# Rows moved directly within SBUF, ahead of inputs and weights, with a later gate for four weight blocks and no empty output products

## The chip, the cores and the metric

The kernel runs on one core of a Trainium2 chip. The metric is the device time of one execution in microseconds (us); lower is better. The engines are TensorE (PE, with its weight loads PEld), VectorE (DVE), ScalarE (ACT), GpSimd (POOL) and SyncE (SP), which here only issues DMA transfers and waits.

## The reference

Three stages run one after the other on 4 batches x 768 tokens:

```
# 1. decaying linear attention, 8 heads of 48, one step per token
scale = minimum(|a|, 0.999) / (|a| + 1e-6);  a_n = a * scale          # a = a_re + i*a_im
S_re, S_im = a_n.re*S_re - a_n.im*S_im + outer(k_t, v_t),  a_n.re*S_im + a_n.im*S_re
y_t = q_t @ S_re
# 2. first network, 384 -> 1536 -> 384, 3072 tokens
xn = x / rms(x) * rms_g;   x1 = (silu(xn @ w_gate) * (xn @ w_val)) @ w_out
# 3. second network, 384 -> 2048 -> 384
out = softplus(x1 @ w_in) @ w_out2
```

## The kernel before

**Units and tiles.** The attention is cut into 24 units of 128 tokens. For unit n, ACT and DVE prepare decay factors, scaled keys and scaled queries (the steps named in `DVE_PREP`, from "t" to "Q") and write them into `pk`, which holds 384 rows (head and channel) as three blocks of 128 partitions, for the real and imaginary plane. The last of these DVE steps is "Q". TensorE needs the same rows in `mm`: partition = plane x channel (96), then head. The networks work on tiles of 512 tokens, four units each; there are six.

**From `pk` to `mm`.** A row of 257 numbers changes its partition on the way, so it goes through DRAM: `store_pk(n)` (L352) waits for step "Q" of unit n and writes all of `pk` to `rows_scratch`; `load_mm(m, hf)` (L345) waits for the store and reads four heads (half `hf`) back in two DMAs, one for each plane. Then `decay` (L1066, DVE) and `kt_of`, `scores`, `outputs` (PE) use them. `pk` is a single buffer: `decay_column(n)` on DVE, its first writer, waits until unit n-1 has left it.

**Three stages in time.** In the *lead* (units 0 to 5) no network runs. SP, ACT, DVE and PE each have a function `lead`, called once for each unit n: DVE prepares n, while the attention of unit m = n-1 and the norm of unit x = n-2 run beside it. Two of the first network's twelve weight blocks are also loaded in each: SP loads three slabs at a time into `ytile` (`load_w1`, L358), ACT writes a rounded copy and its negative (`w1_hi`, L647 and L649), POOL adds the original by an accumulating DMA (`w1_lo`, L518). Then the *first network* runs, six tiles of four steps; each step has three blocks of gate, value and output products on PE (L1488) and, beside them, the attention of one unit and the preparation of another. From unit 24 on there is nothing to prepare. The *second network* is products alone, with ACT and DVE for softplus.

**What sets the order.** Each engine runs its instructions in the order of the code, and only semaphores tie engines together. SP's order in the lead is: the a-input of unit n+1, values and rows of unit m, first weight block, keys and queries of n, second weight block, store of n:

```
load_a(n + 1)                     # waits for DVE step "an" of n
load_v(m); load_mm(m, 0, 1 - par); load_mm(m, 1, 1 - par)
load_w1(w1[0]); load_kq(n); load_w1(w1[1])
store_pk(n, par)                  # waits for DVE step "Q" of n
```

The a-input feeds `front_sq(n+1)` (ACT, L575), which comes in ACT's `lead(n)` after `products_by_row(n)`, and whose result `sum_of(n+1)` (DVE, L886) adds; that DVE instruction stands in `lead(n)` right after `after_sums(n, 1)`, ahead of the rest of unit n's own preparation. `load_v(m)` and the rows of half 1 wait until the attention of unit m-1 has used the buffers (`ys_done[1]`), the rows of half 0 for `ys_done[0]`.

Between lead and first tile PE waits for `y_copied`, `s_added`, all 36 `w_hi` and all 36 `w_lo`, and runs three products of a zero operand into `ybank` (L1636) that open an accumulation. The output products of a tile's last two blocks are put off into the next tile (`spill`), so tile 0 begins with two spills of a tile that doesn't exist: their operand is zero.

Of the kernel before, what the change touches and what calls it, by code (L numbers as in the profile page):

```python
# [18 lines left out]
F32 = mybir.dt.float32  # L19
F32R = mybir.dt.float32r  # L20
I32 = mybir.dt.int32
ALU = mybir.AluOpType
# [3 lines left out]
P = 128  # L26
B, H, S, D = 4, 8, 768, 48
DM = H * D
# [12 lines left out]
HH = H // 2  # L41
ROW = 2 * CH + 1
LEAD = 6
LAG = 1

SUM_LIMIT = -2000.0
# [83 lines left out]
def program(nc, a_d, kq_d, v_d, w1_d, w2_d, g_d, fa_d, fv_d, out_d):  # L130
    ctx = ExitStack()
    with ctx:
# [6 lines left out]
        def sem(name):  # L139
            return ctx.enter_context(nc.semaphore(name))  # L140


        rows_d = nc.dram_tensor("rows_scratch", (2, 2, DM, ROW), F32, kind="Internal").ap()
        y_d = nc.dram_tensor("y_scratch", (NT + 1, P, NJ, TOK), F32, kind="Internal").ap()

        x_d = nc.dram_tensor("x_scratch", (UNITS_B, BK, NBK, NE * B * H * EQ), F32, kind="Internal").ap()
# [70 lines left out]
        const_gp, const_ready = sem("const_gp"), sem("const_ready")  # L217
        gain_in, mask_out, mask_in = sem("gain_in"), sem("mask_out"), sem("mask_in")
        a_loaded, kq_loaded, v_loaded = sem("a_loaded"), sem("kq_loaded"), sem("v_loaded")
        pk_stored, mm_loaded = sem("pk_stored"), [sem(f"mm_loaded{i}") for i in range(2)]  # L220
        afront, aprep = Stage(sem("act_front"), ACT_FRONT), Stage(sem("act_prep"), ACT_PREP)
        s_done = sem("s_done")
        dprep = Stage(sem("dve_prep"), DVE_PREP)
# [3 lines left out]
        ys_done, y_copied, s_added, decayed = [sem(f"ys_done{i}") for i in range(2)], sem("y_copied"), sem("s_added"), sem("decayed")  # L227
        xt_done, xh_done, xl_done = sem("xt_done"), sem("xh_done"), sem("xl_done")
        w_loaded = [sem(f"w_loaded{i}") for i in range(3)]
        w_hi, w_neg, w_lo = sem("w_hi"), sem("w_neg"), sem("w_lo")  # L230
        w2_loaded = [sem(f"w2_loaded{i}") for i in range(3)]
        w2_hi, w2_lo = sem("w2_hi"), sem("w2_lo")
        gv_done, silu_done, p_done = sem("gv_done"), sem("silu_done"), sem("p_done")
# [87 lines left out]
        def _(sp):  # L321
# [16 lines left out]
                after((ys_done[1], m))  # L338
                sp.dma_start(v_in[:, :, :], v_d[m]).then_inc(v_loaded, 16)

            def load_mm(m, hf, par):
                after((pk_stored, 16 * (m + 1)), (ys_done[hf], m))
                heads = slice(hf * HH, (hf + 1) * HH)
                for z in range(2):
                    sp.dma_start(mm[z * D:(z + 1) * D, heads, :],  # L345
                                 rows_d[par, z].rearrange("(h d) c -> d h c", d=D)[:, heads, :]).then_inc(
                                     mm_loaded[hf], 16)

            def store_pk(n, par):

                after((dprep.sem, dprep.at("Q", n)))
                sp.dma_start(rows_d[par].rearrange("z (j p) c -> p z j c", p=P), pk[:, :, :, :]).then_inc(pk_stored, 16)  # L352

            def load_w1(f):
                for kind in range(3):
# [11 lines left out]
                    sp.dma_start(stage2[:, i, :], w2_d[f, kind]).then_inc(w2_loaded[i], 16)  # L367

            def lead(n, m, par, w1):
                load_a(n + 1)  # L370
                if m is not None:
                    load_v(m)
                    load_mm(m, 0, 1 - par)
                    load_mm(m, 1, 1 - par)
                load_w1(w1[0])
                load_kq(n)
                load_w1(w1[1])
                store_pk(n, par)

            def step(n, m, par):  # L380
                if m is not None:
                    load_v(m)
                    load_mm(m, 0, 1 - par)
                if n is not None and not (isinstance(n, int) and n + 1 >= NU):
                    load_a(n + 1)
                if m is not None:
                    load_mm(m, 1, 1 - par)
                if n is not None:
                    load_kq(n)
                if n is not None:  # L390
                    store_pk(n, par)

            def store_y(T):
                after((y_act, 2 * (T + 1)), (y_dve, T + 1))
# [87 lines left out]
        def _(pool):  # L482
# [32 lines left out]
            def w1_lo(f):  # L515
                for kind in range(3):
                    pool.wait_ge(w_neg, 3 * f + kind + 4)
                    pool.dma_start(slab[:, 6 * f + 2 * kind + 1, :], w1_d[f, kind],  # L518
                                   accum_op=ALU.add).then_inc(w_lo, 16)

            def w2_lo_of(slot):
                q0 = sum(len(x) for x in W2_PLAN[:slot])
# [351 lines left out]
        def _(dve):  # L874
# [129 lines left out]
                tt(scaled[:, :, :], frame[:, :, :], gv[:, :].unsqueeze(1).broadcast_to([P, 2, NJ]), ALU.mult, "Cim", n)  # L1004

            def decay_column(n):
                need(dve, pk_stored, 16 * n)
                tick(dve.tensor_copy(pk[:, :, :, 2 * CH], carry[:, :].unsqueeze(1).broadcast_to([P, 2, NJ])))

            def last_products(n):  # L1010
# [49 lines left out]
                return pk[:, z, :, first:first + CH].rearrange("p j (i b) -> p j i b", i=BK)  # L1060

            def decay(m, hf):
                dve.wait_ge(mm_loaded[hf], 32 * (m + 1))
                need(dve, s_added, 2 * m + hf - 1)
                heads = slice(hf * HH, (hf + 1) * HH)
                dve.tensor_tensor(state[:, heads, :], state[:, heads, :],  # L1066
                                  mm[:, heads, 2 * CH:2 * CH + 1].broadcast_to([2 * D, HH, D]), ALU.mult).then_inc(decayed, 1)
# [416 lines left out]
        def _(pe):  # L1484
# [4 lines left out]
                return last  # L1489

            def kt_of(m, hf):
                pe.wait_ge(mm_loaded[hf], 32 * (m + 1))
                need(pe, y_copied, 2 * m + hf)
                need(pe, s_added, 2 * m + hf)
                for h in range(HH):
                    last = pe.transpose(xbank[:, h * 2 * D:(h + 1) * 2 * D], mm[:, hf * HH + h, 0:CH],  # L1496
                                        ident[0:2 * D, 0:2 * D])
                last.then_inc(kt_done, 1)
# [31 lines left out]

            def gate_val(T, f, par, kind):
                g = 2 * f + kind
                if kind == 0:
                    pe.wait_ge(p_done, F1 * T + f)
                else:
                    need(pe, silu_done, F1 * T + f + 1)
                for k in range(NJ):
                    last = split_product(gbank[g % 3][:, :], 6 * f + 2 * kind, slice(k * P, (k + 1) * P),
                                         xh[:, par, k, :], xl[:, par, k, :], k == 0, k == NJ - 1)
                last.then_inc(gv_done, 1)  # L1540
# [19 lines left out]
                last.then_inc(out_done, 1)  # L1560

            def out_block(T, f):
                if f < 2:
                    spill(T, f)
                else:
                    out_of(T, f - 2, f == 2, False)
# [35 lines left out]
            def lead(m, x):  # L1602
# [4 lines left out]
                        last = pe.transpose(lead_xt[:, j * CH:(j + 1) * CH], xn[:, j * P:(j + 1) * P], ident[:, :])  # L1607
                    last.then_inc(xt_done, 1)
                for hf in range(2):
                    pe.wait_ge(mm_loaded[hf], 32 * (m + 1))  # L1610
                    need(pe, y_copied, 2 * m - 1 + hf)
                    need(pe, s_added, 2 * m - 1 + hf)
                    for h in range(HH):
                        last = pe.transpose(lead_bank[hf][:, h * 2 * D:(h + 1) * 2 * D], mm[:, hf * HH + h, 0:CH],
                                            ident[0:2 * D, 0:2 * D])
                    last.then_inc(kt_done, 1)
                    need(pe, masked, 2 * m - 1 + hf)
                    for h in range(HH):
                        last = pe.matmul(lead_scores[hf][:, h * CH:(h + 1) * CH], mm[:, hf * HH + h, 0:CH],
                                         mm[:, hf * HH + h, CH:2 * CH], start=True, stop=True)  # L1620
                    last.then_inc(sc_done, 1)
# [6 lines left out]
                lead(m, m - 1)  # L1628
            pe.wait_ge(y_copied, 2 * (LEAD - 1))
            pe.wait_ge(s_added, 2 * (LEAD - 1))  # L1630
            pe.wait_ge(w_hi, 3 * F1)
            pe.wait_ge(w_lo, 16 * 3 * F1)
            pe.wait_ge(silu_done, 1)

            for m in range(NJ):
                pe.matmul(ybank[m][:, :], slab[:, 0, 0:P], ph[:, 0, :], start=True, stop=False)  # L1636
            for T in range(NT):
                tile(T, T % 2)

# [92 lines left out]


CONSTS = 17
W1_LEAD = [(2 * n, 2 * n + 1) for n in range(LEAD)]
W2_RANK = [i for slot in W2_PLAN for i in range(len(slot))]

# [43 lines left out]
```

## Time and profile before

| | |
|---|---|
| Three runs | 1174.2 us median (1171.81 to 1175.09) |
| Profiled execution | 1175.1 us; span from first to last instruction 1173.4 us |
| PE / DVE / ACT / POOL busy | 1074.7 / 701.8 / 679.3 / 290.2 us |
| Lead, up to the store of unit 5 | 0 to 148.9 us |
| First network from its first product | 156.5 to about 766 us |
| DMA moved | 98.15 MB |

In the profile, a line such as L345 is that of kernel.py. "Idle before, releaser" is how long an engine stood still ahead of an instruction and what ended it. SPq rows are DMA issues: the start is when SP began to issue, the duration is that of the issue, and the time to landing is told separately.

### The profile page before, as it was taken

How to read it: one execution, taken by the hardware profiler on the slowest of the kernel's cores; microseconds unless marked ns; L12 is line 12 of the kernel's file. 1: busy time of each engine (PE TensorE's matmuls, PEld its weight loads, DVE VectorE, ACT ScalarE, POOL GpSimd, SP SyncE). 2: the span in 40 equal slices, each digit the busy share in tenths (PEclk: the TensorE clock that was granted, in tenths of full speed). 3: DMA queues.
4: the chain of work that ended last, by engine and by line, in shares of the span. 5: the costliest groups of instructions: out<-in, count | busy, mean ns of one | idle time of the engine just before them, and what ended most of it. 6: DMA issues, size and time to landing. Idle time of an engine off the chain costs nothing.

```text
span 1173.4 us, 17259 instructions
## 1 busy us (share of the span) xinstructions
PE 1074.7 (92%) x5495; PEld 913.2 (78%) x5495; DVE 701.8 (60%) x2227; ACT 679.3 (58%) x1217; POOL 290.2 (25%) x260
## 2 busy tenths in 40 slices
PE   0456689999999999999999999989999999999997
PEld 0456678888888888888888878878888888888886
DVE  7798959999999999999999211212221313122211
ACT  5566646555555565665554333466666667676664
POOL 2211211111111111111111116733333333333332
PEclk9999999999999999999999999989999999999999
DMA  4988853433343443334332303320100101010000
GB/s 114 208 206 216 189 128 88 115 89 88 89 137 100 106 132 107 88 88 116 88 89 75 101 1 122 119 70 1 52 3 1 55 0 54 0 54 0 27 1 28
DMA packets 69051, 98.15 MB, mean 84 GB/s; under 512 B 5232, under 2 KB 58864, under 8 KB 68976
## 3 DMA queue, kind: packets, MB, share of 16 engines
q1 hardware_dynamic: 63792, 90.15, 27.0%
q0 software_dynamic: 5184, 7.08, 3.9%
q8 instruction: 38, 0.62, 0.2%
q14 instruction: 37, 0.30, 0.1%
HBM read 67.97 MB, written 29.24 MB: 83 GB/s over the span
## 4 chain that ended last, share of the span: by engine, by line
PE 34%; issue 26%; DVE 11%; DMA 11%; POOL 10%; ACT 6%; SPq 1%; POOLq 0%; DVEq 0%; ACTq 0%
PE gbank L1488 16%; POOL pl L556 10%; PE ybank L1488 10%; DMA rows_scratch<-pk 5%; DMA mm<-rows_scratch 4%; DVE prep L882 3%; PE sbank L1505 2%; DVE pk L882 2%; PE xbank L1517 2%; PE xbank L1516 1%; PE xbank L1520 1%; ACT L730 1%; PE xbank L1496 1%; DMA ytile<-in_w 1%; DVE state L1066 1%
## 5 line engine op out<-in xcount | busy, mean ns | idle before, releaser
L1488 PE MATMUL gbank<-xh,slab 128*128 128x512 f32 x1296 | 404.3, 393 | 1.5 <-ACT xh L641 1.5
L1488 PE MATMUL ybank<-ph,slab 128*128 128x512 f32 x1020 | 319.6, 395 | 4.8 <-ACT ytile L678 3.9
L1488 PEld LDWEIGHTS gbank<-xh,slab 128*128 128x128 f32 x1296 | 241.5, 189 | 50.2 <-ACT xh L641 1.7
L1488 PE MATMUL gbank<-xl,slab 128*128 128x512 f32 x648 | 253.3, 391 | 0.0
L1488 PEld LDWEIGHTS ybank<-ph,slab 128*128 128x128 f32 x1020 | 189.3, 189 | 42.9 <-issue 5.6
L531 POOL TENSOR_TENSOR pl<-hid,ph 128x512 fp32r<-128x512 f32 x72 | 99.7, 1384 | 461.4 <-ACT ph L671 461.4
L1488 PE MATMUL ybank<-pl,slab 128*128 128x512 f32 x510 | 199.6, 391 | 0.0
L556 POOL TENSOR_TENSOR pl<-hid,ph 128x512 fp32r<-128x512 f32 x96 | 125.6, 1309 | 268.0 <-ACT ph L817 268.0
L1368 DVE SCALAR_TENSOR_TENSOR hid<-gbank,hid 128x512 f32<-128x512 f32 x72 | 49.7, 691 | 214.4 <-ACT hid L808 214.4
L1488 PEld LDWEIGHTS gbank<-xl,slab 128*128 128x128 f32 x648 | 122.0, 188 | 26.2
L1488 PEld LDWEIGHTS ybank<-pl,slab 128*128 128x128 f32 x510 | 96.2, 189 | 20.8
L671 ACT ACTIVATE ph<-hid 128x512 fp32r<-128x512 f32 x72 | 45.8, 637 | 105.7 <-PE ybank L1488 100.9
L1136 DVE TENSOR_TENSOR hid<-gbank,hid 128x512 f32<-128x512 f32 x72 | 49.4, 686 | 90.1 <-PE gbank L1488 90.0
L817 ACT ACTIVATE ph<-hid 128x512 fp32r<-128x512 f32 x96 | 60.6, 631 | 72.4 <-DVE hid L1368 70.3
L882 DVE TENSOR_TENSOR prep<-prep 128x384 f32<-128x384 f32 (+2 forms) x264 | 88.9, 367 | 1.7
L1516 PE MATMUL xbank<-v_in,at 128*128 128x48 f32 x344 | 68.7, 283 | 8.1 <-issue 6.6
L1517 PE MATMUL xbank<-state,mm 96*128 96x48 f32 x344 | 71.3, 291 | 0.0
L808 ACT ACTIVATE hid<-hid,one 128x512 f32<-128x512 f32 x96 | 69.4, 723 | 3.2
L666 ACT ACTIVATE hid<-gbank 128x512 f32<-128x512 f32 x72 | 42.7, 592 | 44.0 <-PE gbank L1488 43.1
L1516 PEld LDWEIGHTS xbank<-v_in,at 128*128 128x128 f32 x344 | 58.2, 207 | 11.0 <-issue 9.4
L804 ACT ACTIVATE hid<-gbank 128x512 f32<-128x512 f32 x72 | 43.0, 597 | 39.6 <-PE gbank L1488 39.6
L1368 DVE SCALAR_TENSOR_TENSOR hid<-xbank,hid 128x512 f32<-128x512 f32 x24 | 16.6, 692 | 81.8 <-ACT hid L808 81.8
(155 smaller groups left out, 1604.0 us busy)
## 6 DMA issues: line engine op xcount, KB each, us to landing
rows_scratch<-pk SPq DMA_DIRECT2D x24, 771.0 KB, 4.9
mm<-rows_scratch SPq DMA_DIRECT2D x96, 192.8 KB, 4.5
a_in<-in_a SPq DMA_DIRECT2D x24, 384.0 KB, 4.9
kq_in<-in_kq SPq DMA_DIRECT2D x24, 384.0 KB, 5.9
ytile<-in_w SPq DMA_DIRECT2D x36, 192.0 KB, 4.7
slab<-in_w POOLq DMA_DIRECT2D x36, 192.0 KB, 5.7
prep<-in_w SPq DMA_DIRECT2D x32, 192.0 KB, 2.5
y_scratch<-ytile SPq DMA_DIRECT2D x7, 768.0 KB, 5.4
```

Source lines behind the costliest of these rows:

```text
L531: pool.tensor_tensor(pl[:, f % 2, :], hid[:, f % 2, :], ph[:, f % 2, :].bitcast(F32), ALU.subtract).then_inc(lo_done, 1)
L556: pool.tensor_tensor(pl[:, f % 2, :], hid[:, f % 2, :], ph[:, f % 2, :].bitcast(F32), ALU.subtract).then_inc(lo2_done, 1)
L671: act.activation(ph[:, f % 2, :], hid[:, f % 2, :], ACT.Copy).then_inc(hi_done, 1)
L804: act.activation(hid[:, f % 2, :], hbank[f % 4][:, :], ACT.Abs).then_inc(abs_done, 1)
L808: act.activation(hid[:, f % 2, :], hid[:, f % 2, :], ACT.Ln, bias=one[:, 0:1]).then_inc(l_done, 1)
L817: act.activation(ph[:, f % 2, :], hid[:, f % 2, :], ACT.Copy).then_inc(hi2_done, 1)
L882: tick(dve.tensor_tensor(out, a, b, op))
L1136: dve.tensor_tensor(hid[:, f % 2, :], gbank[(2 * f + 1) % 3][:, :], hid[:, f % 2, :], ALU.mult).then_inc(p_done, 1)
L1368: dve.scalar_tensor_tensor(out=hid[:, f % 2, :], in0=hbank[f % 4][:, :], scalar=0.0, in1=hid[:, f % 2, :], op0=ALU.max, op1=ALU.add).then_ ...
L1488: last = pe.matmul(out, slab[:, slot + part, cols], x, start=f, stop=l)
L1516: pe.matmul(bank[:, h * D:(h + 1) * D], at[:, h, :], v_in[:, head, :], start=True, stop=False)
L1517: pe.matmul(bank[:, h * D:(h + 1) * D], mm[:, head, CH:2 * CH], state[:, head, :], start=False, stop=True)
```

## The change

`rows_scratch`, `store_pk` and `load_mm` are gone. `move_rows(m, hf)` copies straight from `pk` to `mm` within SBUF. A head's 48 rows lie in one or two of `pk`'s blocks, so a half has five pieces (heads 2 and 5 have two each), and with two planes ten DMAs, 20 for a unit. In the lead the moves, which wait for step "Q" of unit n-1, stand ahead of the a-input of unit n+1 and the weights; in a tile's step they take the place of the loads. `decay_column` waits for both halves' moves of the unit before. PE waits for 24 `w_hi` and `w_lo` (eight blocks) before tile 0, and for the others at block 8 of tile 0. The zero products now end their accumulation, they signal `out_done` by 2, and the two spills of tile 0 are left out.

```
+EARLY = 8
-            def load_mm(m, hf, par):
-                after((pk_stored, 16 * (m + 1)), (ys_done[hf], m))
-                heads = slice(hf * HH, (hf + 1) * HH)
+            def move_rows(m, hf):
+                after((dprep.sem, dprep.at("Q", m)), (ys_done[hf], m))
                 for z in range(2):
-                    sp.dma_start(mm[z * D:(z + 1) * D, heads, :],
-                                 rows_d[par, z].rearrange("(h d) c -> d h c", d=D)[:, heads, :]).then_inc(
-                                     mm_loaded[hf], 16)
-            def store_pk(n, par):
-                after((dprep.sem, dprep.at("Q", n)))
-                sp.dma_start(rows_d[par].rearrange("z (j p) c -> p z j c", p=P), pk[:, :, :, :]).then_inc(pk_stored, 16)
+                    for h, d, j, p, rows in PIECES[hf]:
+                        sp.dma_start(mm[z * D + d:z * D + d + rows, h, :], pk[p:p + rows, z, j, :]).then_inc(mm_loaded[hf], 16)
...
             def lead(n, m, par, w1):
+                if m is not None:
+                    move_rows(m, 0)
+                    load_v(m)
+                    move_rows(m, 1)
                 load_a(n + 1)
-                if m is not None:
-                    load_v(m)
-                    load_mm(m, 0, 1 - par)
-                    load_mm(m, 1, 1 - par)
                 load_w1(w1[0])
                 load_kq(n)
                 load_w1(w1[1])
-                store_pk(n, par)
             def step(n, m, par):
                 if m is not None:
                     load_v(m)
-                    load_mm(m, 0, 1 - par)
+                    move_rows(m, 0)
                 if n is not None and not (isinstance(n, int) and n + 1 >= NU):
                     load_a(n + 1)
                 if m is not None:
-                    load_mm(m, 1, 1 - par)
+                    move_rows(m, 1)
                 if n is not None:
                     load_kq(n)
-                if n is not None:
-                    store_pk(n, par)
...
             def decay_column(n):
-                need(dve, pk_stored, 16 * n)
+                need(dve, mm_loaded[0], MOVED * n)
+                need(dve, mm_loaded[1], MOVED * n)
...
             def gate_val(T, f, par, kind):
+                if T == 0 and f == EARLY and kind == 0:
+                    pe.wait_ge(w_hi, 3 * F1)
+                    pe.wait_ge(w_lo_late, 16 * 3 * (F1 - EARLY))
             def out_block(T, f):
+                if T == 0 and f < 2:
+                    return
...
-            pe.wait_ge(w_hi, 3 * F1)
-            pe.wait_ge(w_lo, 16 * 3 * F1)
+            pe.wait_ge(w_hi, 3 * EARLY)
+            pe.wait_ge(w_lo, 16 * 3 * EARLY)
             for m in range(NJ):
-                pe.matmul(ybank[m][:, :], slab[:, 0, 0:P], ph[:, 0, :], start=True, stop=False)
+                last = pe.matmul(ybank[m][:, :], slab[:, 0, 0:P], ph[:, 0, :], start=True, stop=True)
+            last.then_inc(out_done, 2)
...
+def pieces(hf):
+    out = []
+    for h in range(hf * HH, (hf + 1) * HH):
+        d = 0
+        while d < D:
+            c = h * D + d
+            rows = min(D - d, P - c % P)
+            out.append((h, d, c // P, c % P, rows))
+            d += rows
+    return out
+PIECES = [pieces(hf) for hf in range(2)]
+MOVED = 16 * 2 * len(PIECES[0])
```

## Rows read from the trace of the kernel before

**Rows 1.** Windows: stretch, length, busy us (instructions) of each engine, clock, DMA share, GB/s
```profile
126.04:148.91 22.87, 15.53 (x77) 14.73 (x77) 21.49 (x84) 15.02 (x33) 4.71 (x6) 1.00 0.89 213
...
370.00:477.00 107.00, 105.63 (x625) 90.79 (x624) 102.43 (x350) 62.54 (x118) 16.98 (x12) 1.00 0.38 104
```

**Rows 2.** Timeline of SP, lead and tile 0: start, duration, queue, line, destination<-source, count
```profile
21.30 2.26 SPq L358 DMA_DIRECT2D ytile<-in_w x3
27.96 0.39 SPq L352 DMA_DIRECT2D rows_scratch<-pk  x1
28.39 5.30 SPq L421 DMA_DIRECT2D causal<-mask_scratch  x8
...
52.93 0.38 SPq L352 DMA_DIRECT2D rows_scratch<-pk  x1
...
101.60 0.38 SPq L352 DMA_DIRECT2D rows_scratch<-pk  x1
106.58 0.33 SPq L330 DMA_DIRECT2D a_in<-in_a  x1
...
107.53 2.07 SPq L345 DMA_DIRECT2D mm<-rows_scratch  x4
...
126.04 0.38 SPq L352 DMA_DIRECT2D rows_scratch<-pk  x1
...
130.62 0.33 SPq L339 DMA_DIRECT2D v_in<-in_v  x1
...
148.91 0.38 SPq L352 DMA_DIRECT2D rows_scratch<-pk  x1
...
188.24 0.39 SPq L352 DMA_DIRECT2D rows_scratch<-pk  x1
```

**Rows 3.** Source view of L345 (ns min/median/max); DMA view, 28 to 157 us
```profile
L345 SPq DMA_DIRECT2D mm<-rows_scratch x96: 303/410/550, 35.0 to 650.9; - x96
...
a_in<-in_a SPq DMA_DIRECT2D x5, 384.0 KB, 4.6
```

**Rows 4.** Waits of DVE, 28 to 149 us: total, times, longest
```profile
DVE prep L910 <- ACT prep L593: 6.7, 4, 2.5
DVE state L1066 <- DMA mm<-rows_scratch: 4.6, 7, 1.0
```

**Rows 5.** Timelines of DVE and ACT in the lead, around the sum
```profile
110.86 0.84 ACT L575 ACTIVATE front<-a_in 128x768 f32<-128x768 f32 x1 [0.89 <-DMA a_in<-in_a]
...
112.62 0.55 DVE L886 TENSOR_TENSOR front<-front 128x384 f32<-128x384 f32 x1
...
135.54 0.55 DVE L886 TENSOR_TENSOR front<-front 128x384 f32<-128x384 f32 x1
```

**Rows 6.** Timelines of DVE and PE where the first tile begins
```profile
153.86 0.35 DVE L1079 TENSOR_TENSOR state<-gbank,state 96x192 f32<-96x192 f32 x1 [1.88 <-ACT xnat L690]
...
156.52 1.62 PE L1636 MATMUL ybank<-ph,slab 128*128 128x512 f32 x3 [3.06 <-DMA slab<-in_w]
...
160.50 1.05 PE L1488 MATMUL gbank<-xh,slab 128*128 128x512 f32 x2
...
163.14 0.62 PE L1488 MATMUL gbank<-xh,slab 128*128 128x512 f32 x2
...
164.09 0.69 DVE L1136 TENSOR_TENSOR hid<-gbank,hid 128x512 f32<-128x512 f32 x1 [9.41 <-PE gbank L1488]
```

**Rows 7.** Chain of waits: start, duration, what (one block of output products)
```profile
182.09 2.08 PE ybank L1488 x9
```

**Rows 8.** Timelines of DVE and PE in a step of the first network
```profile
415.23 0.56 DVE L886 TENSOR_TENSOR front<-front 128x384 f32<-128x384 f32 x1 [0.30 <-ACT front L575]
...
421.76 0.52 PE L1496 MATMUL xbank<-ident,mm 96*128 96x96 f32 x4 [0.19 <-DVE state L1101]
```

**Rows 9.** Waits of PE, 157 to 690 us
```profile
PE xbank L1496 <- DVE state L1101: 4.0, 11, 0.7
...
PE xbank L1496 <- DMA mm<-rows_scratch: 2.4, 5, 0.9
```

More of the change, by code:

```diff
@@ L140, in sem @@
             return ctx.enter_context(nc.semaphore(name))
-        rows_d = nc.dram_tensor("rows_scratch", (2, 2, DM, ROW), F32, kind="Internal").ap()
         y_d = nc.dram_tensor("y_scratch", (NT + 1, P, NJ, TOK), F32, kind="Internal").ap()
@@ L219, in program @@
         a_loaded, kq_loaded, v_loaded = sem("a_loaded"), sem("kq_loaded"), sem("v_loaded")
-        pk_stored, mm_loaded = sem("pk_stored"), [sem(f"mm_loaded{i}") for i in range(2)]
+        mm_loaded = [sem(f"mm_loaded{i}") for i in range(2)]
         afront, aprep = Stage(sem("act_front"), ACT_FRONT), Stage(sem("act_prep"), ACT_PREP)
@@ L229, in program @@
         w_loaded = [sem(f"w_loaded{i}") for i in range(3)]
-        w_hi, w_neg, w_lo = sem("w_hi"), sem("w_neg"), sem("w_lo")
+        w_hi, w_neg, w_lo, w_lo_late = sem("w_hi"), sem("w_neg"), sem("w_lo"), sem("w_lo_late")
         w2_loaded = [sem(f"w2_loaded{i}") for i in range(3)]
@@ L518, in w1_lo @@
                     pool.dma_start(slab[:, 6 * f + 2 * kind + 1, :], w1_d[f, kind],
-                                   accum_op=ALU.add).then_inc(w_lo, 16)
+                                   accum_op=ALU.add).then_inc(w_lo if f < EARLY else w_lo_late, 16)
             def w2_lo_of(slot):
@@ L1062, in decay @@
             def decay(m, hf):
-                dve.wait_ge(mm_loaded[hf], 32 * (m + 1))
+                dve.wait_ge(mm_loaded[hf], MOVED * (m + 1))
                 need(dve, s_added, 2 * m + hf - 1)
@@ L1491, in kt_of @@
             def kt_of(m, hf):
-                pe.wait_ge(mm_loaded[hf], 32 * (m + 1))
+                pe.wait_ge(mm_loaded[hf], MOVED * (m + 1))
                 need(pe, y_copied, 2 * m + hf)
@@ L1609, in lead @@
                 for hf in range(2):
-                    pe.wait_ge(mm_loaded[hf], 32 * (m + 1))
+                    pe.wait_ge(mm_loaded[hf], MOVED * (m + 1))
                     need(pe, y_copied, 2 * m - 1 + hf)
```

## The prediction

> **What bounds the kernel now.** I read the windows first, to cut the run into stages, then for each stage the timeline of the engine that is nearly full, then SP's timeline, because the change is mostly one of SP's order. In the lead DVE is busy 21.5 of 22.9 us of a unit while PE has 15.5 and the DMA share is 0.89; in the first network DVE has 102.4 and PE 105.6 of 107 us [rows 1]. So in the lead the time is DVE's list plus what DVE stands still for; in the first network DVE and PE hold each other, and neither has 5% to give.
>
> The length of a lead unit is the distance between two stores, since each store waits for DVE's last step "Q": units 1 to 5 take 148.91 - 27.96 = 120.95 us, and the four from 52.93 on take 95.98, or 24.0 each [rows 2]. In these five units DVE waits 6.7 us for ACT at L910 (ACT is late there because it converts weights first) and 4.6 us for `mm` at L1066 [rows 4]. For the a-input it hardly waits: ACT squares it at 110.86, 9.3 us after the store at 101.60, and DVE adds it at 112.62, 11.0 after that store [rows 2, 5].
>
> **The moves in the lead.** Removed: one store and four loads of a unit. Added: 20 issues on SP, in the same place in time (right after "Q"), and everything that SP issues later in that unit stands behind them. Let Q be the time of the last unit's step "Q". What does an issue cost? L345's median is 0.41 us, 0.30 at the least and 0.55 at most [rows 3]; four in a row take 2.07, 0.52 each, and eight transfers of only 8 KB take 5.30, 0.66 each with one long one among them [rows 2]. So small pieces are not cheaper to issue than large ones. I take 0.445 from one start to the next: the median issue, and a little for the gap between two. The ends that I keep are 0.36 and 0.50.
>
> - Ten moves of half 0: Q to Q+4.45. The values then wait for `ys_done[1]`, which before let them go 4.58 us after the store (130.62 - 126.04) [rows 2]; that is now Q+4.6, and they take 0.35.
> - Ten moves of half 1: Q+4.95 to Q+9.4. Only now is the a-input issued, at Q+9.4. Before it was Q+5.0 (106.58 - 101.60) [rows 2].
> - It lands 4.6 us later, the median of the lead's five [rows 3] (ends 3.5 and 5.8 for other traffic around it): Q+14.0. The square takes 0.84 [rows 5], with the signal 0.9: DVE can add at Q+14.9, where before it added at Q+11.0.
> - From that instruction to the next "Q", DVE needed 148.91 - 135.54 = 13.37 and 126.04 - 112.62 = 13.42 us [rows 2, 5]. Of this the waits for `mm` go away, since the last move is issued by Q+9.4 and even at the 4.6 of a larger transfer has landed by Q+14: 4.6 / 5 = 0.9 each [rows 4]. That leaves 12.5.
>
> A lead unit thus takes 14.9 + 12.5 = 27.4 us against 24.0: four of them 109.6 - 95.98 = **+13.6**. The 6.7 us for ACT at L910 are no gain, as that stall lies ahead of the sum, where DVE now has slack. Unit 1 is reckoned apart. SP's last weight issue before it ends at 23.56; the eight mask loads no longer stand behind a store and take 5.3, to 28.9; moves and values take 9.3, to 38.2; landing, square and the rest give 38.2 + 4.6 + 0.9 + 12.5 = 56.2 for the second "Q", which was at 52.93 [rows 2]: **+3.3**. The lead: **+16.9**. What else is behind the moves has room: keys and queries are issued near Q+11.5 and used some 7 us after the sum, the first weight block is needed after the ACT work that follows the square. DRAM traffic of the rows falls away (0.77 MB each way), and that helps landings, not issues.
>
> With the ends: 0.36 and 3.5 us give an a-input issued at Q+8.6, a sum at Q+13.0 and units of 25.5, so +6.0 in four and nothing in unit 1, **+6**. With 0.50 and 5.8 it is Q+10.4, Q+17.1 and 29.6, +22.4 and some 5 in unit 1, **+28**.
>
> On small transfers the Trainium skill speaks against the change: "DMA: Bandwidth & Descriptors", section "Rules for kernel authors", says to coalesce many small transfers, because under 64 KB one pays mostly overhead. The trace agrees as far as issues go, 0.66 us each for 8 KB against 0.52 for 193 KB [rows 2]. By the page's fit in its section on the SWDGE path (2.0 us plus bytes / 436e3) a piece of 49 KB would be estimated at 2.1 us; if the 20 pieces of a unit ran strictly one after the other, that would be 42 us a unit, longer than a whole step. But the eight 8 KB loads were issued inside 5.3 us, so issues at least overlap what the page puts into one transfer.
>
> **The start of tile 0.** PE waited 3.06 us for the last weight slab and began at 156.52 [rows 6]. The new gate of eight blocks is long open; what is late next is the state add at 153.86 + 0.35 = 154.2 [rows 6], 5.3 us after the last "Q" of the lead. That is **-2.3**, if the clock follows. The trace has two matmuls in 1.05 us at 160.50 and in 0.62 at 163.14 [rows 6]: PE started the tile at the lower of its two levels (1.2 GHz) and had the upper one some 5 us of unbroken work later. If the rise stays where it is in time and doesn't move with the start, the first products take longer and the gain is 0.8. I take -2.2. The last four blocks are awaited at block 8, more than two steps later, and four steps take 107 us [rows 1], so by then they have been there for about 50; this wait costs nothing and has nothing behind it.
>
> **No empty products.** PE loses 18 products and their weight loads; nine take 2.08 [rows 7], so that is 4.1 us of PE work, half of it directly after the first value product. But from 164.09, where that value product is ready, to the next "Q" at 188.24 [rows 2, 6] DVE needs 24.1 us, and its timeline shows it at work nearly without a break. The attention outputs need DVE's mask, and the keys of half 1 need its state add. PE, now earlier, will wait there instead: what was a product becomes a wait. I take **0**, with -4.1 as the other end.
>
> **The moves in the tiles.** A step is a ring: PE to ACT, ACT's square to DVE's sum (waited 0.30 at 415.23), DVE's state add to PE's keys (waited 0.19 at 421.76) [rows 8]. None of it passes through `mm`. The a-input there waits for DVE's "an", which follows the first gate product, so ten moves are through by about the same time; half 1 of the rows and the keys are issued some 2 us later than before, and both are used only near the end of the step. What is gained is at most PE's waits for `mm`, 2.4 us in five places [rows 9], some of which DVE (4.0 in eleven) takes over. I take **-1**, between -2.4 and 0. If this cover failed, each microsecond would count 18 times; half a microsecond each would be +9, inside the range. The wait in `decay_column` stands behind `decay(m, 1)`, which already waits for the same moves: nothing.
>
> **Sum.** +16.9 - 2.2 + 0 - 1 = +13.7. The profiled execution took 1175.1 us (span 1173.4 and 1.7 around it), so 1188.8; it lies 0.9 above the median of the three runs, against which the same sum gives 1187.9. I say **1188**. Its own range, from the ends, is +6 - 2.3 - 2.4 = +1 to +28 - 0.8 = +27 at the extremes, 1176 to 1202; both ends of every term together are unlikely.
>
> **Rivals.**
> - *Faster: the a-input is not late.* The five DVE waits for `mm` (4.6 us) and the start (2.2) are gained, and some of the empty products: -8 or so, **1166**. For it speaks that these waits stand in the profile, and that the rows' way is one transfer shorter. It decides at DVE's sum in the lead: for a unit no longer than 24.0 us the sum must come by Q+11.5 and the a-input be issued by Q+6, so 20 issues must take less than 5.5 us, under 0.28 each. The least of 96 issues is 0.30 [rows 3]. 12%.
> - *Near no change:* cheap issues and quick landings, with all of the gains at the start and at `mm`: +1, **1175.5**. 12%.
> - *The empty products count in full*, because PE and not DVE sets tile 0: 13.7 - 4.1, **1184**. Against it is DVE's full list there. 12%.
> - *The moves are slow as transfers too*, so that the a-input queues behind them: +27, **1202**. For it: DMA share 0.89 in the lead [rows 1]. Against: half of the rows' traffic goes away. 10%.
> - *The pieces run one after the other*, 2 us or so each, as the rule above would have it at its worst: 42 us a unit instead of 24 and 27, some +350 us, near **1520**. The eight mask loads speak against it. 2%.
> - The forecast: 52%.
>
> Slower by over 0.3% is the forecast, the third, fourth and fifth rivals and a little of the second: 0.77. Within 0.3% (3.5 us, about what these measurements can tell from no change) 0.10, faster 0.13. For eight in ten I take 1175 to 1200.
>
> **What would show it.** In the changed kernel's lead DVE should wait at L886 (the sum) for ACT, about 5 us for each of units 1 to 5, and ACT at the square for the a-input by as much; the waits at L910 matter no more and those for `mm` are gone; SP should show ten issues in about 4.5 us; the distance of two "Q" should be near 27.4. PE should begin tile 0 some 5.3 us after the last lead "Q", then wait for DVE in the first step; steps should stay at 26.7. I am wrong if DVE has no wait at its sum, or if the steps change.

## The result, and the profile of the changed kernel

The changed kernel takes **1202.8 us** (median of four runs, 1201.78 to 1204.25) against 1174.1 (1171.81 to 1175.09): the ratio is **1.0244, 95% interval 1.0226 to 1.0261**. Slower was forecast, but by 13.7 us and not by 28.7, and 1202.8 lies above the range of 1175 to 1200. The profiled execution took 1201.78 us with a span of 1200.0, so the spans differ by 26.6.

First the windows, for they say in which stage the time went. The columns are the stretch and its length, busy us (instructions) of PE, PEld, DVE, ACT and POOL, the granted clock, the DMA share and GB/s. A lead unit, and four steps of the first network, of the changed kernel:

```profile
118.86:148.98 30.12, 15.56 (x77) 14.84 (x77) 21.46 (x84) 15.03 (x33) 5.39 (x7) 1.00 0.58 137
401.00:508.00 107.00, 105.94 (x626) 90.81 (x624) 102.53 (x350) 62.45 (x119) 17.00 (x12) 1.00 0.26 75
```

Beside [rows 1] the same 84 instructions of DVE take the same 21.5 us in a lead unit, but the unit is 30.1 us long instead of 22.9 (over the five units 30.2 on average instead of 24.2). The DMA share fell from 0.89 to 0.58, so the lead got slower with less traffic. Four steps still fill 107 us. (The clock column reads 1.00 in the lead, but two of the attention's small matmuls take 0.63 us there, and 0.39 at 199.82 in the first step. So PE is at its lower level in the lead, in the kernel before too; there DVE and not PE sets the time.) Cut at the end of DVE's step "Q", the whole difference comes out as follows:

| Stretch | before | after | difference |
|---|---|---|---|
| Q of unit 0 to Q of unit 5 (five lead units) | 121.0 | 151.0 | +30.0 |
| to the next Q (the first tile begins in it) | 39.3 | 38.2 | -1.1 |
| the next 16 steps | 429.7 | 428.8 | -0.9 |
| the rest | 555.5 | 554.1 | -1.4 |

So the lead lost 30.0 us. The reason stands on SP's timeline (start, duration of the issues, queue, line, destination<-source, count):

```profile
88.88 6.23 SPq L345 DMA_DIRECT2D mm<-pk  x10
95.16 0.58 SPq L339 DMA_DIRECT2D v_in<-in_v  x1
95.83 6.22 SPq L345 DMA_DIRECT2D mm<-pk  x10
102.10 0.58 SPq L330 DMA_DIRECT2D a_in<-in_a  x1
...
118.86 6.27 SPq L345 DMA_DIRECT2D mm<-pk  x10
```

Ten moves start at Q (88.88), the values follow at once, and then ten more. From the first move to the values is 6.28 us, 0.63 for each issue. The a-input is issued 13.2 us after Q, where it was 5.0 before [rows 2]. What follows from it stands on ACT and DVE:

```profile
105.41 0.84 ACT L565 ACTIVATE front<-a_in 128x768 f32<-128x768 f32 x1 [8.25 <-DMA a_in<-in_a]
...
106.38 0.56 DVE L876 TENSOR_TENSOR front<-front 128x384 f32<-128x384 f32 x1 [6.48 <-ACT front L565]
```

ACT has stood still for 8.25 us when the a-input is there, and DVE for 6.48 when it may add. That add comes 17.5 us after Q, where it was 11.0 [rows 5], and the next Q is 118.86 - 106.38 = 12.5 us later. DVE's waits from 28 to 165 us (total, times, longest):

```profile
DVE front L876 <- ACT front L565: 30.8, 4, 8.6
DVE prep L900 <- ACT prep L583: 4.0, 5, 1.5
```

The waits for `mm` of [rows 4] are gone, those at the line that was L910 went from 6.7 to 4.0, and the new wait at the sum is 30.8 us in four of the five units (with the fifth, up to 179 us, 38.2).

The other place is the start of tile 0. PE's timeline (the number in brackets is how long PE had stood still, and for whom):

```profile
184.33 1.62 PE L1632 MATMUL ybank<-ph,slab 128*128 128x512 f32 x3 [0.85 <-ACT xnat L680]
...
199.82 0.39 PE L1507 MATMUL xbank<-v_in,at 128*128 128x48 f32 x2 [3.64 <-DVE at L1082]
...
204.74 1.05 PE L1479 MATMUL gbank<-xh,slab 128*128 128x512 f32 x2
...
208.30 0.62 PE L1479 MATMUL gbank<-xh,slab 128*128 128x512 f32 x2
```

PE begins 184.33 - 178.9 = 5.4 us after the last Q of the lead, as forecast (before: 156.52 - 148.91 = 7.6 [rows 6]). The 3.06 us for the weight slab are gone. But nine of the 18 empty products stood right ahead of the attention output (the other nine some 7 us earlier), and there PE now stands still for 3.64 us, waiting for DVE's mask. From 201 until about 208 us two matmuls take 1.05 us instead of the 0.62 that they take at the end, and DVE has to wait for one of the gate products among them. DVE's wait, and the window (columns as above):

```profile
209.95 0.69 DVE L1127 TENSOR_TENSOR hid<-gbank,hid 128x512 f32<-128x512 f32 x1 [2.03 <-PE gbank L1479]
```

```profile
199.50:210.00 10.50, 10.18 (x46) 8.86 (x47) 8.37 (x46) 5.94 (x10) 1.29 (x1) 0.67 0.16 48
```

The granted clock was 0.67 there, a mix of the two levels, 1.2 and 2.4 GHz. DVE is busy 8.37 of the 10.50 us.

### The profile page after: what moved, and what is told of

Its sections match the earlier page's. It is cut to its first block, busy times and chain, and to the rows that moved or that the text cites. A ratio compares the mean times of both kernels' runs of the same rounds, so it can differ in the third digit from the quotient of the medians.

```text
span 1200.0 us, 17585 instructions
## 1 busy us (share of the span) xinstructions
PE 1071.9 (89%) x5477; PEld 912.3 (76%) x5477; DVE 701.5 (58%) x2227; ACT 678.2 (57%) x1217; POOL 290.8 (24%) x260
## 3 DMA queue, kind: packets, MB, share of 16 engines
q1 hardware_dynamic: 51120, 71.22, 19.7%
## 4 chain that ended last, share of the span: by engine, by line
PE 35%; issue 27%; DVE 10%; POOL 10%; ACT 10%; DMA 5%; SPq 2%; POOLq 0%; DVEq 0%; ACTq 0%
PE gbank L1479 17%; POOL pl L546 10%; PE ybank L1479 10%; DVE prep L872 3%; DMA ytile<-in_w 3%; SPq L345 2%; PE xbank L1508 2%; PE xbank L1507 2%; DMA a_in<-in_a 2%; PE sbank L1496 2%; ACT L720 2%; ACT front L565 2%; PE xbank L1511 1%; ACT prep L599 1%; PE xbank L1487 1%
## 5 line engine op out<-in xcount | busy, mean ns | idle before, releaser
L1479 PE MATMUL ybank<-ph,slab 128*128 128x512 f32 x1008 | 315.9, 395 | 4.8 <-ACT ytile L668 3.9
L1479 PE MATMUL ybank<-pl,slab 128*128 128x512 f32 x504 | 197.0, 391 | 0.0
L1479 PEld LDWEIGHTS gbank<-xl,slab 128*128 128x128 f32 x648 | 122.3, 189 | 26.2
L508 POOL DMA_DIRECT2D slab<-in_w x36 | 30.9, 860 | 148.2 <-ACT slab L639 147.1
L794 ACT ACTIVATE hid<-gbank 128x512 f32<-128x512 f32 x72 | 43.0, 597 | 39.6 <-PE gbank L1479 39.6
```

What stands on the lines that cost most here:

```text
L794: act.activation(hid[:, f % 2, :], hbank[f % 4][:, :], ACT.Abs).then_inc(abs_done, 1)
L1479: last = pe.matmul(out, slab[:, slot + part, cols], x, start=f, stop=l)
```

## The experiments

Four kernels at first, beside a kernel before at 1174.43 us. The theory was that the time sits in the lead, because the a-input stands behind twenty slow issues.

**a_between.** The a-input goes out between the two rows of ten; nothing else changes.

```diff
                 if m is not None:
                     move_rows(m, 0)
+                load_a(n + 1)
+                if m is not None:
                     load_v(m)
                     move_rows(m, 1)
-                load_a(n + 1)
```

> The changed kernel with one thing moved: in the lead, SP issues the a-input after the ten moves of half 0 instead of after all twenty. Theory (the lead is long because DVE waits for the a-input, which stands behind twenty issues of 0.62 us): the a-input is issued near Q+6.3 and DVE's sum comes by Q+11; the moves of half 1 end some 0.6 us later, near Q+13.6, so DVE waits 1 to 2 us for them; a lead unit takes 24 to 25 us instead of 30, and the time is 1173 to 1180. Rival (the moves themselves or their transfers slow the lead, wherever the a-input stands): the units stay near 30 and the time at 1200 or more.

Measured: 1183.13 us (1182.96 to 1185.11), ratio 1.0074 (1.0047 to 1.0101). One reordering takes back 19.7 of the 28.7 us. SP and DVE in one unit:

```profile
81.37 6.23 SPq L345 DMA_DIRECT2D mm<-pk  x10
87.64 0.58 SPq L330 DMA_DIRECT2D a_in<-in_a  x1
```

```profile
91.88 0.56 DVE L877 TENSOR_TENSOR front<-front 128x384 f32<-128x384 f32 x1 [0.93 <-ACT front L566]
...
96.46 0.35 DVE L1058 TENSOR_TENSOR state<-state,mm 96x192 f32<-96x192 f32 x1 [2.29 <-DMA mm<-pk]
```

The a-input is issued 6.3 us after Q, the sum comes at Q+10.5, and the wait there shrinks to 0.93. Units are 26.2 to 26.9 us long instead of 29.7 to 31.3. They don't reach 24, since now the second row of moves is late: DVE waits 2.29 us for it, 11.2 us in the five units. A third wait is new, 4.7 us in the five units for the keys and queries: SP issues them 15.3 us after Q as in the changed kernel, but DVE now comes to them sooner. The time is 3 us above the upper end of what I had expected, for I had not reckoned the second wait so high, nor the third at all.

**dram_source.** The same twenty pieces, of the same shape, read from an input in DRAM instead of from `pk`. The attention thus works on wrong rows; the order of the work is unchanged.

```diff
-  sp.dma_start(mm[...], pk[p:p + rows, z, j, :])
+  sp.dma_start(mm[...], kq_d[m][p:p + rows, z, 0:ROW])
```

> The changed kernel, but each of the twenty pieces of a unit is read from rows of the key input in DRAM, of the same count, length and partitions, instead of from pk; so the attention works on wrong rows, and only the time counts. Theory A (an issue costs 0.62 us instead of 0.45 because both ends are in SBUF): issues fall to about 0.45, lead units to about 27, the time to about 1187. Theory B (a row of ten small issues costs 0.62 each whatever the source): issues and units stay as they are, time 1200 to 1205.

Measured: 1185.50 us (1183.02 to 1186.93), ratio 1.0088 (1.0060 to 1.0116). SP in one unit:

```profile
81.61 4.55 SPq L345 DMA_DIRECT2D mm<-in_kq  x10
86.21 0.42 SPq L339 DMA_DIRECT2D v_in<-in_v  x1
86.73 4.56 SPq L345 DMA_DIRECT2D mm<-in_kq  x10
91.33 0.42 SPq L330 DMA_DIRECT2D a_in<-in_a  x1
```

The count, the sizes and the destination are the same, only the source is not: ten issues take 4.55 instead of 6.23 us, 0.46 instead of 0.63 from start to start. Units are 25.9 to 27.7, where 27.4 was forecast. With about the issue cost that the forecast had taken (0.46 for 0.445) the unit comes out close to the forecast, 26.7 on average. The issue of the values and of the a-input behind the moves costs 0.42 here too, and 0.58 in the changed kernel.

**a_late.** The kernel before, with the a-input issued behind the four loads of rows. Nothing else of the change is in it, and it has few issues.

```diff
             def lead(n, m, par, w1):
-                load_a(n + 1)
                 if m is not None:
                     load_v(m)
                     load_mm(m, 0, 1 - par)
                     load_mm(m, 1, 1 - par)
+                load_a(n + 1)
```

> The kernel before the change, rows through DRAM, with the a-input of the lead issued after the four loads of rows instead of ahead of them: near Q+8 instead of Q+5. Theory (the place of the a-input sets the unit): DVE's sum comes at about Q+13.5 and units take 26 us instead of 24, so the time is 1182 to 1186. Rival (DVE has slack for the a-input): no change, 1174.

Measured: 1188.12 us (1187.25 to 1189.98), ratio 1.0110 (1.0076 to 1.0145). SP in one unit, and DVE's largest wait from 28 to 165 us:

```profile
90.08 1.78 SPq L345 DMA_DIRECT2D mm<-rows_scratch  x4
91.91 0.44 SPq L330 DMA_DIRECT2D a_in<-in_a  x1
```

```profile
DVE front L886 <- ACT front L575: 22.5, 5, 4.9
```

A late a-input alone, with four issues ahead of it, makes the kernel 13.7 us slower, and it shows in the very wait of the changed kernel. That is what the theory says of the mechanism. The units (26.6 to 28.2) are longer than expected, and the time is 2 us above the range. The clock isn't what makes them so: the column gives 0.59 from 54.5 to 164.6 us here (0.70 in dram_source, 1.00 in the changed kernel), but two of the attention's matmuls take 0.63 us in the lead of all three, and the two executions of a_late with a mean clock of 0.998 took 1187.25 and 1188.49 us.

**empty_kept.** The changed kernel with the 18 empty products put back. They read blocks 0 and 1, which the early gate covers, so that the gate stays early.

```diff
             def out_block(T, f):
-                if T == 0 and f < 2:
-                    return
 ...
```

> The changed kernel with the eighteen empty output products of tile 0 put back (with weight blocks 0 and 1, whose product with zero is the same). Theory (without them PE stands still 3.6 us before the attention outputs of the first step, its clock falls to the lower level and the next products take twice as long, which costs DVE 2 us at its third gate product): PE has no wait there, no matmul in the step runs at the lower level, and the time is about 2 us lower, 1200.8 against 1202.8. Rival (fewer products are a gain or nothing): the time is the same or up to 4 us higher.

Measured: 1201.07 us (1200.98 to 1201.36), ratio 1.0224 (1.0189 to 1.0258): 1.75 us *faster* than without those products, by the medians. The intervals of the two ratios overlap, but the slowest of its four runs is below the fastest of the changed kernel's (1201.78). PE at the places of the third fence of the result:

```profile
200.57 0.32 PE L1507 MATMUL xbank<-v_in,at 128*128 128x48 f32 x2
...
203.73 0.62 PE L1479 MATMUL gbank<-xh,slab 128*128 128x512 f32 x2
```

and the same window:

```profile
199.50:210.00 10.50, 9.82 (x64) 8.45 (x63) 10.07 (x49) 8.03 (x14) 1.29 (x1) 1.00 0.17 51
```

There is no wait ahead of the output, the clock is 1.00, and the two matmuls take 0.62. PE gets through 64 instructions in the 10.5 us instead of 46. The stretch from the last Q of the lead to the next one is 36.3 us instead of 38.2.

The other kernels bear this out. From DVE's first gate product to the next Q it takes 24.1 or 24.2 us in all eight that keep the products, with a clock of 1.00 in these 10.5 us of the step. In the four that leave them out (the changed kernel, a_between, dram_source, hybrid_no_empty) PE waits 3.64 or 3.65 us ahead of the output, the clock is 0.54 to 0.67, and the stretch takes 26.1 to 27.1 us.

The second set asks whether there is a version that keeps the gains and not the cost. It stands beside a kernel before at 1175.04 us.

**gate_only.** The kernel before with the later gate for the last four blocks alone; the empty products stay and read blocks 0 and 1.

```diff
-            pe.wait_ge(w_hi, 3 * F1)
-            pe.wait_ge(w_lo, 16 * 3 * F1)
+            pe.wait_ge(w_hi, 3 * EARLY)
+            pe.wait_ge(w_lo, 16 * 3 * EARLY)
...
+                if T == 0 and f == EARLY and kind == 0:
+                    pe.wait_ge(w_hi, 3 * F1)
+                    pe.wait_ge(w_lo_late, 16 * 3 * (F1 - EARLY))
```

> The kernel before the change with only the late gate for the last four weight blocks (the empty products stay, with blocks 0 and 1). Theory: TensorE begins tile 0 about 5 us after the lead's last Q instead of 7.5, nothing else moves, and the time falls by 2 to 3 us, to about 1172. Rival (the clock rises later or DVE is late anyway): no change, 1174.

Measured: 1171.87 us (1168.68 to 1175.21), ratio 0.9977 (0.9964 to 0.9991). PE begins the tile 5.4 us after the last Q (148.87), 2.2 earlier than in [rows 6]:

```profile
154.30 1.62 PE L1640 MATMUL ybank<-ph,slab 128*128 128x512 f32 x3 [0.85 <-ACT xnat L691]
...
157.98 0.63 PE L1489 MATMUL gbank<-xh,slab 128*128 128x512 f32 x2
```

Two matmuls take 0.63 us already at 157.98, 3.7 after PE's start; before they took 1.05 still at 160.50, 4.0 after it, and had had a wait of 3.06 us ahead [rows 6]. So the clock rises sooner too. From that Q to the next it takes 36.2 us instead of 39.3: the 2.2 of the earlier start and about 0.9 on top.

**tiles_direct.** The kernel before with the direct moves in the tile steps only; the lead keeps its way through DRAM.

```diff
             def lead(n, m, par, w1):
 ...
-                store_pk(n, par)
+                if n < LEAD - 1:
+                    store_pk(n, par)
             def step(n, m, par):
 ...
-                    load_mm(m, 0, 1 - par)
+                    move_rows(m, 0)
```

> The kernel before the change with the direct moves in the tiles' steps only; in the lead the rows still go through DRAM. Theory (twenty issues of 0.63 us a unit fit beside a step of 26.7 us, and mm is there a little earlier): the distance of two Qs stays at 26.7 and the time is 0 to 2.5 us lower, 1172 to 1174. Rival (half 1 or the keys come late in the steps): steps grow, 1178 or more.

Measured: 1171.97 us (1168.94 to 1175.06), ratio 0.9978 (0.9967 to 0.9990). PE's waits in the tiles, 157 to 690 us:

```profile
PE xbank L1505 <- DVE state L1110: 5.9, 17, 0.8
```

The 2.4 us for `mm` of [rows 9] are gone, and DVE has taken over a part of them, 5.9 us where it was 4.0. The 16 steps take 428.8 us instead of 429.7, and the stretch ahead of them 37.7 instead of 39.3.

**hybrid.** Both together: gate_only's edits and those of tiles_direct.

> Both of these together: rows through DRAM in the lead, direct in the tiles, late gate, empty products kept. If the parts add: 4 to 5 us below the kernel before, 1169.5, with lead units at 24. If the gain at the start is taken back by DVE in the first steps: 1172 to 1174.

Measured: **1171.29 us** (1167.99 to 1172.99), ratio **0.9972 (0.9961 to 0.9983)**. It beats both kernels: 0.3% under the one before, 2.6% under the changed one. Its last lead unit, with the 21.6 us of DVE's work and the high DMA share of [rows 1], is 24 us long and not 30:

```profile
123.33:147.29 23.96, 15.60 (x77) 14.80 (x77) 21.58 (x84) 15.14 (x33) 5.73 (x7) 1.00 0.91 208
```

The two parts gained 3.2 and 3.1 us alone and 3.75 together, which leaves hybrid about 2 us above what I had expected. In the profiles both shorten the same stretch: the one that holds the last lead Q to the next (36.2 and 37.7 us alone, 36.6 together, 39.3 before). So they overlap there, and by the intervals hybrid isn't shown to be faster than either part alone.

**act_a.** The changed kernel, but ACT issues the a-input of the lead, so no move is ahead of it. Two things more differ: on SP the keys and queries go ahead of the first weight block, and the empty products are kept.

```diff
             def lead(n, m, par, w1):
 ...
                     move_rows(m, 1)
-                load_a(n + 1)
-                load_w1(w1[0])
                 load_kq(n)
+                load_w1(w1[0])
 # in ACT's list, after the middle of unit n
+                act.dma_start(a_in[:, :, :], a_d[n + 1]).then_inc(a_loaded, 16)
```

> The changed kernel with the a-input of the lead issued by ACT right after its step that waits for the same DVE step, the keys ahead of the weights on SP, and the empty products kept; all twenty moves stay where the change put them. Theory (of the moves only their being ahead of the a-input costs time): lead units fall from 30 to 24.5 to 26, bounded by the last of twenty moves at Q+12.8 plus 2 us of landing, and the time is 1170 to 1178. Rival (twenty issues cost the lead 6 us a unit however the a-input comes): units near 30, 1200.

Measured: 1175.57 us (1174.17 to 1176.35), ratio 1.0004 (0.9991 to 1.0017). SP in one unit of the lead, and DVE at the state's decay in it:

```profile
102.84 6.24 SPq L345 DMA_DIRECT2D mm<-pk  x10
109.80 6.23 SPq L345 DMA_DIRECT2D mm<-pk  x10
```

```profile
118.19 0.35 DVE L1057 TENSOR_TENSOR state<-state,mm 96x192 f32<-96x192 f32 x1 [2.48 <-DMA mm<-pk]
```

SP issues the same twenty dear moves, at the same price, and the time is 27.3 us below the changed kernel's, of which the empty products are some 1.8 (empty_kept). So it was not the moves that cost most of the time, but that the a-input stood behind them; a_between shows the same with the a-input's place alone, where here the keys moved too. The units are 24.5 to 25.9 us, and the lead takes 126.5 us where it was 121.0: what is left is that the last of the twenty moves is late (9.5 us of waits in four units). The gains behind the lead make up for it.

The last two ran beside a kernel before at 1175.42 us.

**store_split.** The kernel before with its one store cut into six of 128 rows each, so that the issue of a piece from SBUF to DRAM can be read.

```diff
-                sp.dma_start(rows_d[par].rearrange("z (j p) c -> p z j c", p=P), pk[:, :, :, :]).then_inc(pk_stored, 16)
+                for z in range(2):
+                    for j in range(NJ):
+                        sp.dma_start(rows_d[par][z, j * P:(j + 1) * P, :], pk[:, z, j, :]).then_inc(pk_stored, 16)
```

> The kernel before the change with the store of a unit's rows cut into six (one for each plane and block of 128 partitions), to measure one thing, the distance of two issues in a row whose source is SBUF and whose destination is DRAM. Theory A (reading from SBUF makes an issue dear): 0.63 us, as for the moves. Theory B (only SBUF at both ends does): 0.46 us, as for loads from DRAM. The time is some 2 to 3 us a lead unit higher in A and 1.5 to 2 in B, as the loads wait for the last store.

Measured: 1195.47 us, a single run. SP:

```profile
28.20 2.79 SPq L354 DMA_DIRECT2D rows_scratch<-pk  x6
```

Six issues in 2.79 us are 0.47 each: with the source in SBUF and the destination in DRAM an issue costs about what it does the other way round. Of the kinds tried, only pieces with both ends in SBUF cost 0.63. The lead's five units grew by 4.3 us, 0.9 each and not the 1.5 to 2 expected. The run is 20 us slower all the same, which I had not expected, because the rows arrive later in every tile step: from 240 to 600 us PE waits 13.4 us for `mm` in 13 places, where it was 1.6 in 4, and 16 steps take 444.4 us instead of 429.7, 27.8 each instead of 26.9. SP issues the rows' loads 1.2 to 1.7 us later after Q, so their way through DRAM has less than a microsecond of room in a tile step.

**hybrid_no_empty.** hybrid with the empty products taken out.

> The hybrid (rows through DRAM in the lead, direct in the tiles, late gate) with the eighteen empty products of tile 0 left out too. Theory (without them TensorE stands still before the first attention outputs and falls to the lower clock): a wait of 3 to 4 us there, matmuls at half speed after it, the distance from the lead's last Q to the next 1 to 2 us longer than the hybrid's 36.6, and the time 1172 to 1173. Rival (4.1 us less work for TensorE is a gain once the lead is short): 1168 to 1170.

Measured: 1174.04 us (1170.39 to 1176.18), ratio 0.9982 (0.9966 to 0.9997). PE:

```profile
171.63 0.63 PE L1526 MATMUL xbank<-v_in,at 128*128 128x48 f32 x2 [3.65 <-DVE at L1101]
...
177.74 1.05 PE L1498 MATMUL gbank<-xh,slab 128*128 128x512 f32 x2
...
181.04 0.62 PE L1498 MATMUL gbank<-xh,slab 128*128 128x512 f32 x2
```

The same wait of 3.65 us and the same matmuls at the lower level appear in a kernel whose lead is not slow, and the stretch from Q to Q is 39.6 us instead of 36.6. So it is the missing products and nothing else of the change that brings them. In the profile it is 3 us; by the ratios, with hybrid's beside it, 0.001 or 1.2 us, and those intervals overlap. The sign is borne out by two pairs of kernels and by the stretch of all twelve profiles; what it is worth in the time of the whole kernel, 1 to 3 us, isn't settled.

## Why the prediction was right and wrong

**The mechanism was right.** DVE waits for ACT at its sum, ACT for the a-input, the next Q is 12.5 us after the sum (12.5 forecast), the steps kept their length, and a_between and a_late move the time by moving the a-input alone. The size was half of what came.

**The step that failed is the cost of an issue in "the moves in the lead".** The text asked "What does an issue cost?" and took 0.445 us, with 0.36 and 0.50 as its ends. It measured 0.63, above the upper end. The a-input was thereby issued at Q+13.2 and not at Q+9.4, +3.8 us a unit. Its landing was quicker than taken, 3.4 us (median of the lead's five) for 4.6: -1.2. That the rows' traffic had halved doesn't explain it, for in act_a, with the same moves, the a-input takes 4.6 again. The sum so came at Q+17.5 for Q+14.9. The four units from the second Q on took 30.3 on average for 27.4, +11.7, and the second Q itself came at 57.6 for 56.2, +1.4: that is the missing 13.1 us of the lead (+30.0 for +16.9). The rows that I took the price from [rows 3] have one end in DRAM, as all transfers of SP in that profile. For a transfer with both ends in SBUF the trace of before had no row, and the ends of the range were those of a different kind of transfer. I named the 0.66 for each of eight mask loads [rows 2] and then left it outside the range. It would have given the right number, but by luck. The same eight loads in the changed kernel:

```profile
23.59 3.87 SPq L411 DMA_DIRECT2D causal<-mask_scratch  x8
```

That is 0.48 each, so a small size alone doesn't make an issue dear, and the prediction's reading that 8 KB cost more to issue than 193 KB doesn't hold.

**Where SBUF lies at both ends, and not how many rows a piece has**, decides the price. Pieces of 16, 32 and 48 rows had issues of 0.59 us each (medians) in the changed kernel, and dram_source kept the pieces and changed the source.

**The start of tile 0** was forecast as -2.2. From the last Q to PE's first product it gained 2.2 (7.6 to 5.4), and gate_only shows it by itself. DVE's first gate product came 12.0 us after Q, where it was 15.2: 3.2, because the clock came up sooner too: two matmuls took the full 1.05 us for the last time at 185.75, 1.4 us after PE's start, where it was 4.0 after it before. The end of the term that said the rise might stay where it is in time was wrong; it moved forward by more than the start.

**The empty products** were forecast as 0 with -4.1 as the other end, and the text said "what was a product becomes a wait". The wait came (3.64 us for 4.1 us of products), and the text stopped there. A wait is not as good as a product: after it PE's matmuls took 1.05 for 0.62 us, and from the first gate product to the next Q it took 26.1 us for 24.1. The term is about +2 in the profile, outside its range on the other side. The Trainium skill, "TensorE: Matmul & The Clock Gate", section "What's actually happening", has the idle array at the lower of its two levels; the trace agrees (0.67 after the wait, 1.00 with the products in its place). I had used the clock for the start of the tile, and not for this step.

**The moves in the tiles** were forecast as -1 and brought -0.9 in the 16 steps. The cover named there held: ten dear issues in a row cost nothing where the a-input waits for DVE anyway.

**The terms together.** Measured by spans: the lead +30.0 (forecast +16.9), the start of tile 0 -3.2 (-2.2), the empty products +2.0 (0), the steps -0.9 (-1), and -1.4 that no term had: +26.5 of the 26.6. The misses outside the lead (-1.0, +2.0, +0.1 and -1.4) nearly cancel, and the time is wrong because of the lead.

**Rivals.** "The moves are slow as transfers too" gave 1202, the time that came, by a cause that did not: a move lands in 2.0 us (median; 2.2 in the lead), the a-input in 3.4, less than the 4.6 of [rows 3], and ahead of the a-input the moves are late as issues. The faster rival fell with its own condition, 20 issues under 5.5 us; they took 12.6. "Near no change" wanted cheap issues as well. "The empty products count in full" fell with the wait for DVE. "The pieces run one after the other" is out: they overlap. On the issues, the Trainium skill says under "DMA: Bandwidth & Descriptors", section "Issuing engines are not separate DMA queues", that the cost on the issuing engine is usually small beside the DMA itself. Each issue here is (0.63 against 2.0); twenty in a row ahead of one awaited load are not.

**Open.** Why an issue with both ends in SBUF is dearer isn't settled: no run here looks inside an issue. The rest of the kernel behind the 16 steps was 553.9 to 554.6 us in the changed kernel, a_between, gate_only, tiles_direct, hybrid and hybrid_no_empty, 555.1 to 555.6 in the kernel before, empty_kept, dram_source, a_late and act_a, and 556.9 in store_split. So -1.4 of the +26.6 is no term of the forecast, and no run explains it.

## What to carry to other kernels

Before a few large transfers are traded for many small ones, count what stands behind them in the same issuing queue and who waits for the first thing behind: issues times their pitch is the delay, even if every transfer is short. Put the awaited load ahead, or on another engine's queue, as a_between and act_a do. And where the trace has no row for a kind of transfer (here with both ends in SBUF), the spread of the kinds that it does show is no range for the price: leave the range open, or measure that one transfer first. Work of an engine that is removed where another one must be waited for anyway gained nothing here, and cost the clock.

## What the runs showed of the hardware

- SP issues one transfer each 0.63 us where both ends are in SBUF, and each 0.46 or 0.47 us where one is in DRAM, from DRAM to SBUF (dram_source) or the other way (store_split). The number of rows, 16 to 48, made no difference (0.59 us an issue in the changed kernel). A load issued right behind a row of such moves cost 0.58 and not 0.33 to 0.43 [rows 2]; behind the moves from DRAM it cost 0.42.
- A move of 48 KB within SBUF landed in 2.0 us (median). The page of the changed kernel (issues, KB of one, us to landing):

```profile
mm<-pk SPq DMA_DIRECT2D x288, 48.2 KB, 2.0
a_in<-in_a SPq DMA_DIRECT2D x24, 384.0 KB, 3.3
```

- 3.6 us without a product were followed by a granted clock of 0.54 to 0.67 over some 10.5 us, in all four kernels that had that wait, and by 7 us of matmuls at the lower of the two levels (201 to 208 us) in the changed kernel, 9 in hybrid_no_empty. With 18 products of no use in that place it stayed at 1.00, in eight kernels.
- The clock column can read 1.00 where the matmuls show the lower level: in the lead it does, with 0.63 us for two small matmuls that take 0.39 later.
